# Order of TensorE's work in the even tiles of the attention blocks

## The chip, the cores and the metric

The kernel runs on one core of one Trainium2 chip. The metric is the device time of one execution in microseconds (us). Times come from repeated runs; the trace comes from one further execution, profiled by the hardware.

## What is computed

Three layers follow each other. Sparse attention: 2 batches, 8 heads, 576 tokens, head dimension 64, the softmax taken over the 32 largest scores of each row. A feed-forward layer on the 1152 tokens (model width 512, hidden width 2048) with a leaky ReLU whose slope is learned. A mixture of 8 experts, of which each token takes the best two.

```python
scores = scale * np.matmul(q, k.transpose(0, 1, 3, 2))
kth = np.partition(scores, -top_k, axis=-1)[..., -top_k:-top_k + 1]
attn = exp(where(scores >= kth, scores, -1e9) - max);  attn /= sum(attn)
x = np.matmul(attn, v)                                   # -> [1152, 512]
h = x @ w_in;  g = np.maximum(h, 0.0) + alpha * np.minimum(h, 0.0);  x2 = g @ w_out
# then gates, top 2 of 8 experts, and per expert relu(x2 @ w1[e]) @ w2[e]
```

## The kernel before

All is float32 in accuracy: large products are made of a high and a low part of each operand (`_high`, `_low`, `_parts`), so a product takes two or three passes of TensorE.

The 1152 tokens are cut in 9 **blocks** of 128 rows. A block has 8 **tiles**, one for each head h. Attention and feed-forward layer run together, as a pipeline over the tiles: while TensorE transposes the probabilities of tile h of block blk, it computes the scores of the tile 5 ahead (AHEAD), works on the feed-forward layer of block blk-1 (`mlp`) and finishes that of block blk-2 (`rest`). The feed-forward layer goes in 4 chunks of 512 hidden columns, chunk c of block j. `first_layer` makes a chunk of h in bank `ps_h`; ScalarE copies it to `h_sb` (`copy_h1`); TensorE turns it (`h_transpose`, four 128x128 transposes into `ps_t`); ScalarE takes the two ReLUs from `ps_t` (`relu_both`), GpSimd puts them together (`prelu`), ScalarE and GpSimd cut the result in a high and a low part (`high_g`, `low_g`), and `second_layer` multiplies it with w_out, 12 matmuls, into `ps_y`.

Each engine runs its own instruction list in order, and the lists are written by hand; semaphores are the only link. TensorE's list is made by `one_block`. Which tile does what is in small tables: `FIRST_AT` (first layer at h = 1, 3, 5, 7), `TURN_AT` (chunks 0, 1, 2 turned at h = 2, 4, 6), `REST_TURN_AT` (chunk 3 at h = 0 of the next block), `SECOND_AT` (chunk 0 at h = 6) and `REST_SECOND_AT` (chunks 1, 2, 3 at h = 0, 2, 4 of the next block). Turns and second layers thus lie in even tiles only.

What the functions of TensorE wait for:
- `prob_transpose` (L889, matmuls L896 and L898): GpSimd's masked probabilities, and ScalarE having emptied the banks.
- `score_tile` (L874, L865): the queries and that ScalarE has copied the scores of the tile before. In block 4 (MIXED), which holds rows of both batches, a tile's scores take 8 matmuls and not 4.
- `h_transpose` (L944, L952): `copy_h1` of its chunk (`act_h1`), and that `ps_t` is free.
- `prob_values` (L900, L912): `copy_prob_t` of this tile (`act_pt`), ScalarE's copy of the turned probabilities to SBUF. 20 small matmuls.
- `second_layer` (L955, L974): `low_g` of its chunk, which stands in GpSimd's list ahead of the probabilities of the same tile. For chunk 0 (h = 6) it also waits for `copy_x2_t` (`act_x2t`), by which ScalarE empties `ps_y` of the block before.
- `x_transpose` (L916, L921) at h = 1, `x2_transpose` (L979, L984) at h = 5 and `gates` (L987, L992) at h = 6.

ScalarE's list in an even tile is: `copy_h1` (L1251), `copy_prob_t` (L1221, L1222), at h = 6 `copy_x2_t` (L1318), the high parts of queries and g, `copy_scores` (L1161), `relu_both` (L1285, L1287), two exponentials (L1215). At h = 3 and 7 the list ends with `copy_o` (L1240, L1241), which waits for the `prob_values` of that tile; so at h = 0 and 4 `copy_h1` stands behind it.

After the 9 blocks a hand-written tail ends the feed-forward layer of blocks 7 and 8 and the routing, and then the expert phase runs, bound by TensorE, from about 504 us on.

Of the kernel before, what the change touches and what calls it, by code (L numbers as in the profile page):

```python
# [81 lines left out]
TURN_AT, REST_TURN_AT = {2: 0, 4: 1, 6: 2}, {0: 3}  # L82
# [3 lines left out]
SECOND_AT, REST_SECOND_AT = {6: 0}, {0: 1, 2: 2, 4: 3}  # L86
# [20 lines left out]
def chunk_of(j, c):  # L107

    return c if j % 2 == 0 else (c + 2) % CHUNKS


def wait(eng, sem, count):

    if not isinstance(count, int) or count > 0:
        eng.wait_ge(sem, count)


def moe_program(nc, q_in_rows, kt_in, v_in, v_tail, w_in, w_out, alpha, w_gates, noise, w1, w2, w_parts, x2_rows, x_sorted,
                out):
    with ExitStack() as ctx:  # L120
# [59 lines left out]
        def sb1(name, shape, dt=F32):  # L180
            return early.enter_context(nc.sbuf_tensor(name, shape, dt))
# [18 lines left out]
        rest = sb1("rest", [P, 2, SEQ])  # L200
# [660 lines left out]
        def _(pe):  # L861
# [12 lines left out]
            def score_tile(tile, h, blk, b):  # L874

                if h % 4 == 0:
                    pe.wait_ge(q_ready[h // 4], blk + 1)
                if isinstance(blk, int) and blk == 0:
                    keys_ready(0, h)
                wait(pe, act_scores, tile)  # L880
                if isinstance(blk, int) and blk == MIXED:
                    b, head = h // PAIRS, 2 * (h % PAIRS)
                    keys_ready(b, head + 1)
                    score_parts(h, b, head + 1)
                    score_parts(h, b, head, DIM).then_inc(pe_scores, 1)
                else:
                    score_parts(h, b, h).then_inc(pe_scores, 1)

            def prob_transpose(tile, h, blk):  # L889
                pe.wait_ge(pool_prob, tile + 1)  # L890
                wait(pe, act_pt, tile)
                if h == 0:
                    wait(pe, act_gate, blk - 2)
                for kt in range(KT):
                    if kt < KT - 1:
                        pe.transpose(ps_pt[:, kt * P:(kt + 1) * P], expo[:, h % 4, kt * P:(kt + 1) * P], ident[:, :])  # L896
                    else:
                        pe.transpose(ps_pt4[0:LASTK, 0:P], expo[:, h % 4, kt * P:SEQ], ident[:, :]).then_inc(pe_pt, 1)  # L898

            def prob_values(tile, h, blk, mixed_block, b):  # L900

                pe.wait_ge(act_pt, tile + 1)
                if h % 4 == 0:
                    wait(pe, act_o, 2 * blk + h // 4)
                if mixed_block and h >= PAIRS:
                    pe.wait_ge(v_in_second[h - PAIRS], 48)
                c = (h % 4) * VCOLS
                heads = (2 * (h % PAIRS), 2 * (h % PAIRS) + 1) if mixed_block else (h, h)
                for kt in range(KT):
                    n = P if kt < KT - 1 else LASTK  # L910
                    for lo, hi, head in ((0, DIM, heads[0]), (DIM, P, heads[1])):
                        mm = pe.matmul(ps_o[lo:hi, c:c + VCOLS], prob_t[0:n, h % 2, kt * P + lo:kt * P + hi],  # L912
                                       v[0:n, head, kt, :], start=(kt == 0), stop=(kt == KT - 1))
                mm.then_inc(pe_pv, 1)

            def x_transpose(j):  # L916
                pe.wait_ge(pool_x, 2 * j + 2)

                wait(pe, act_relu, 4 * j)
                for k in range(MK):  # L920
                    mm = pe.transpose(ps_t[:, k * P:(k + 1) * P], xf[:, k * P:(k + 1) * P], ident[:, :])  # L921
                mm.then_inc(pe_xt, 1)

            def first_layer(j, c, dst=ps_h[:, :], alone=False):
                if j == 0:
                    pe.wait_ge(pool_w_in_low, 2 * c + 2)
                elif c >= 2:
                    pe.wait_ge(w_in_back[c % 2], 16 * j)
                if c == 0:
                    pe.wait_ge(act_xt, j + 1)  # L930
                if not alone:
                    wait(pe, act_h1, 4 * j + c)
                for k in range(MK):
                    for b in range(2):
                        pe.matmul(dst, x_t[:, 0, k, :], w_in_parts[:, c % 2, b, k * 512:(k + 1) * 512],  # L935
                                  start=(k == 0 and b == 0), stop=False)
                if c == 0:
                    pe.wait_ge(dve_xt, j + 1)
                for k in range(MK):
                    mm = pe.matmul(dst, x_t[:, 1, k, :], w_in_parts[:, c % 2, 0, k * 512:(k + 1) * 512],  # L940
                                   start=False, stop=(k == MK - 1))
                mm.then_inc(pe_first, 1)

            def h_transpose(j, c, dst=ps_t, src=h_sb[:, :], banks=1):  # L944
                pe.wait_ge(act_h1, 4 * j + c + 1)

                if c == 0:
                    pe.wait_ge(dve_xt, j + 1)
                else:
                    pe.wait_ge(act_relu, 4 * j + c + 1 - banks)  # L950
                for k in range(4):
                    mm = pe.transpose(dst[:, k * P:(k + 1) * P], src[:, k * P:(k + 1) * P], ident[:, :])  # L952
                mm.then_inc(pe_ht1, 1)

            def second_layer(j, c):  # L955

                last = isinstance(j, int) and j == BLOCKS - 1
                if last:
                    pe.wait_ge(dve_g_low, c + 1)
                else:  # L960
                    pe.wait_ge(pool_g_low, 4 * j + c + 1)
                if j == 0:
                    if c == 2:
                        pe.wait_ge(dve_w_low, 2)
                    else:
                        pe.wait_ge(pool_w_low, (2, 4, 0, 6)[c])
                if c == 0:
                    wait(pe, act_x2, j)
                    if not last:
                        wait(pe, act_x2t, j)  # L970
                for k in range(4):
                    at = slice((4 * chunk_of(j, c) + k) * MODEL, (4 * chunk_of(j, c) + k + 1) * MODEL)
                    for a, w in ((0, w_out_high), (0, w_out_low), (1, w_out_high)):
                        mm = pe.matmul(ps_y[:, :], g_parts[:, c % 2, a, k * P:(k + 1) * P], w[:, at],  # L974
                                       start=(c == 0 and k == 0 and a == 0 and w is w_out_high),
                                       stop=(c == CHUNKS - 1 and k == 3 and a == 1))
                mm.then_inc(pe_second, 1)
# [18 lines left out]
            def one_block(blk, b, mixed_block=False, mlp=True, rest=True, last=False):  # L996
                for h in range(HEADS):
                    tile = HEADS * blk + h
                    prob_transpose(tile, h, blk)
                    if not (last and h + AHEAD >= HEADS):  # L1000
                        score_tile(tile + AHEAD, (h + AHEAD) % HEADS, blk + (h + AHEAD) // HEADS,
                                   1 if mixed_block and h + AHEAD >= HEADS else b)
                    if rest and h in REST_TURN_AT:
                        h_transpose(blk - 2, REST_TURN_AT[h])
                    if mlp and h == 1:
                        x_transpose(blk - 1)
                    if mlp and h in TURN_AT:
                        h_transpose(blk - 1, TURN_AT[h])
                    if h % 2 == 0 or h == 1:
                        prob_values(tile, h, blk, mixed_block, b)  # L1010
                    if mlp and h in FIRST_AT:
                        first_layer(blk - 1, FIRST_AT[h])
                    if mlp and h in SECOND_AT:
                        second_layer(blk - 1, SECOND_AT[h])
                    if rest and h in REST_SECOND_AT:
                        second_layer(blk - 2, REST_SECOND_AT[h])
                    if h % 2 and h != 1:
                        prob_values(tile, h, blk, mixed_block, b)
                    if rest and h == 5:
                        x2_transpose(blk - 2)  # L1020
                    if rest and h == 6:
                        gates(blk - 2)
# [13 lines left out]
            pe.wait_ge(ident_ready, 2)  # L1036
            pe.wait_ge(v_ready, 1)
            one_block(0, 0, mlp=False, rest=False)
            one_block(1, 0, rest=False)
            pe.wait_ge(small_in, 48)  # L1040
# [718 lines left out]
```

## Time and profile before

| | us |
|---|---|
| median of 3 runs | 758.64 |
| lowest and highest of them | 755.74 and 759.49 |
| the profiled execution, whole | 760.67 |
| its span, first to last instruction | 758.9 |

The profiled execution is 2.03 us above the median. In its span block 5 begins at 263.3 us, block 6 at 307.0, block 7 at 350.2 and block 8 at 393.3; a block in the steady part takes about 43.2 us. The trace gives for each instruction or run of like instructions its start and how long it was in flight. Matmuls overlap, so the distance from one start to the next is what an instruction costs TensorE, and its own duration is longer than that. A bracket at the end of a row is idle time of the engine ahead of it and what ended that. The releaser is sometimes named by the tile that another instruction of the same engine wrote.

### The profile page before, as it was taken

How to read it: one execution, taken by the hardware profiler on the slowest of the kernel's cores; microseconds unless marked ns; L12 is line 12 of the kernel's file. 1: busy time of each engine (PE TensorE's matmuls, PEld its weight loads, DVE VectorE, ACT ScalarE, POOL GpSimd, SP SyncE). 2: the span in 40 equal slices, each digit the busy share in tenths (PEclk: the TensorE clock that was granted, in tenths of full speed). 3: DMA queues.
4: the chain of work that ended last, by engine and by line, in shares of the span. 5: the costliest groups of instructions: out<-in, count | busy, mean ns of one | idle time of the engine just before them, and what ended most of it. 6: DMA issues, size and time to landing. Idle time of an engine off the chain costs nothing.

```text
span 758.9 us, 13760 instructions
## 1 busy us (share of the span) xinstructions
PE 664.5 (88%) x4660; PEld 564.7 (74%) x4660; DVE 521.5 (69%) x1103; ACT 465.2 (61%) x878; POOL 392.8 (52%) x435
## 2 busy tenths in 40 slices
PE   2467767999989999999999998369999999999993
PEld 2355656887867888888887777258989989989992
DVE  5799997888779989898989043454555554555520
ACT  5588866777887777777877545614554544535511
POOL 3488899678788677776787634400202202202112
PEclk9987998999999999999999999759999999999998
DMA  9759446643507536244644749380638448366222
GB/s 307 309 185 414 132 167 210 236 169 141 217 17 268 183 127 239 99 192 154 249 140 174 278 182 385 148 291 1 188 118 277 130 160 275 93 213 208 88 32 35
DMA packets 39607, 140.95 MB, mean 186 GB/s; under 512 B 10800, under 2 KB 11824, under 8 KB 35504
## 3 DMA queue, kind: packets, MB, share of 16 engines
q1 hardware_dynamic: 35168, 130.25, 47.5%
q0 software_dynamic: 4384, 9.98, 5.8%
q8 instruction: 32, 0.52, 0.3%
q14 instruction: 23, 0.19, 0.1%
HBM read 113.70 MB, written 45.73 MB: 210 GB/s over the span
## 4 chain that ended last, share of the span: by engine, by line
PE 70%; POOL 11%; DVE 5%; issue 4%; ACT 4%; DMA 4%; POOLq 0%; ACTq 0%; SPq 0%; DVEq 0%
PE bank L1125 12%; PE bank L974 11%; PE ps_scores L1111 9%; PE bank L935 7%; PE bank L1111 6%; PE bank L912 6%; PE bank L1130 4%; PE bank L940 3%; PE ps_scores L865 3%; POOL expo L1567 3%; PE bank L896 3%; DMA q_raw<-q_rows_dram 2%; PE bank L952 2%; DVE top L414 2%; PE bank L1093 1%
## 5 line engine op out<-in xcount | busy, mean ns | idle before, releaser
L1709 POOL DMA_INDIRECT out_dram<-ye,xe x24 | 42.8, 1783 | 219.1 <-ACT ye L1475 214.2
L414 DVE MAX8 top<-rest 128x8 f32<-128x576 f32 x216 | 152.2, 745 | 0.0
L1567 POOL TENSOR_TENSOR expo<-scores,expo 128x576 f32<-128x576 f32 x72 | 103.6, 1440 | 68.1 <-ACT scores L1195 68.0
L426 DVE MATCH_REPLACE8 rest<-top,rest 128x576 f32<-128x576 f32 x144 | 105.7, 741 | 0.0
L974 PE MATMUL bank<-w_out_high,g_parts 128*128 128x512 f32 x288 | 100.2, 410 | 0.0
L1125 PE MATMUL bank<-w_hi,he_t 128*128 128x512 f32 x256 | 91.9, 400 | 0.0
L604 DVE TENSOR_TENSOR w_lo<-raw,w_hi 128x1024 fp32r<-128x1024 f32 x64 | 77.8, 1225 | 19.5 <-ACT w_hi L1419 18.4
L912 PEld LDWEIGHTS bank<-v,prob_t 128*64 128x64 f32 (+1 forms) x1440 | 57.4, 145 | 30.2 <-ACT prob_t L1222 15.6
L912 PE MATMUL bank<-v,prob_t 128*64 128x65 f32 (+1 forms) x1440 | 73.1, 241 | 5.8 <-ACT prob_t L1222 5.8
L414 DVE MAX8 top<-scores 128x8 f32<-128x576 f32 x72 | 52.6, 746 | 33.7 <-ACT scores L1161 33.3
L935 PE MATMUL bank<-w_in_parts,x_t 128*128 128x512 f32 x272 | 71.2, 405 | 2.2 <-DMA w_in_parts<-w_parts_dram 2.2
L896 PE MATMUL bank<-ident,expo 128*128 128x128 f32 x288 | 47.9, 291 | 27.5 <-POOL expo L1567 26.2
L1111 PE MATMUL ps_scores<-xe_t,w_hi 128*128 128x320 f32 x320 | 71.8, 312 | 0.0
L865 PE MATMUL ps_scores<-k_parts,q_high 128*128 128x288 f32 (+1 forms) x160 | 55.4, 361 | 17.9 <-DVE q_low L471 8.1
L1221 ACT ACTIVATE prob_t<-bank 128x512 f32<-128x512 f32 x72 | 43.3, 601 | 43.2 <-PE bank L898 43.1
L1419 ACT CAST w_hi<-raw 128x1024 fp32r<-128x1024 f32 x64 | 66.2, 1044 | 0.2
L974 PEld LDWEIGHTS bank<-w_out_high,g_parts 128*128 128x128 f32 x288 | 54.8, 190 | 13.1
L1468 ACT ACTIVATE he_t<-ps_scores 128x320 fp32r<-128x320 f32 x40 | 17.5, 437 | 76.7 <-PE ps_scores L1111 76.7
L896 PEld LDWEIGHTS bank<-ident,expo 128*128 128x128 f32 x288 | 35.0, 149 | 35.6 <-POOL expo L1567 21.7
L935 PEld LDWEIGHTS bank<-w_in_parts,x_t 128*128 128x128 f32 x272 | 50.1, 192 | 11.9 <-DMA w_in_parts<-w_parts_dram 2.4
L650 DVE SCALAR_TENSOR_TENSOR he_t<-ps_scores,he_t 128x64 fp32r<-128x64 f32 x80 | 22.2, 319 | 53.2 <-ACT he_t L1468 53.2
L1111 PEld LDWEIGHTS ps_scores<-xe_t,w_hi 128*128 128x128 f32 x320 | 55.4, 191 | 2.1
(192 smaller groups left out, 1606.3 us busy)
## 6 DMA issues: line engine op xcount, KB each, us to landing
w_in_parts<-w_parts_dram SPq DMA_DIRECT2D x16, 2048.0 KB, 7.9
raw<-w_dram SPq DMA_DIRECT2D x64, 512.0 KB, 10.8
x_sorted_dram<-x_sorted_dram SPq DMA_DIRECT2D x7, 2570.0 KB, 10.9
w_parts_dram<-w_in_parts SPq DMA_DIRECT2D x4, 2048.0 KB, 10.1
q_raw<-q_rows_dram SPq DMA_DIRECT2D x18, 256.0 KB, 5.0
xe<-x_sorted_dram SPq DMA_DIRECT2D x8, 514.0 KB, 4.6
w_in_raw<-w_in_dram SPq DMA_DIRECT2D x4, 1024.0 KB, 11.0
w_out_raw<-w_out_dram SPq DMA_DIRECT2D x4, 1024.0 KB, 15.8
```

Source lines behind the costliest of these rows:

```text
L414: nc.vector.max(dst, src).then_inc(chain if r < ROUNDS - 1 else dve_top, 1)
L426: nc.vector.match_replace(rest[:, k, :], top[:, (n + k) % 4, 8 * r:8 * r + 8], src, LOWEST).then_inc(chain, 1)
L604: nc.vector.tensor_tensor(w_lo[par][:, at], raw[par][:, at], w_hi[par][:, at].bitcast(F32), ALU.subtract).then_inc(dve_wl, 1)
L865: mm = pe.matmul(ps_scores[0:to, n, 0:HALF], part[:, n_q, 0:to], k_parts[:, k_slot(b, h), n * HALF:(n + 1) * HALF], start=(a == 0), stop=( ...
L896: pe.transpose(ps_pt[:, kt * P:(kt + 1) * P], expo[:, h % 4, kt * P:(kt + 1) * P], ident[:, :])
L912: mm = pe.matmul(ps_o[lo:hi, c:c + VCOLS], prob_t[0:n, h % 2, kt * P + lo:kt * P + hi], v[0:n, head, kt, :], start=(kt == 0), stop=(kt == ...
L935: pe.matmul(dst, x_t[:, 0, k, :], w_in_parts[:, c % 2, b, k * 512:(k + 1) * 512], start=(k == 0 and b == 0), stop=False)
L974: mm = pe.matmul(ps_y[:, :], g_parts[:, c % 2, a, k * P:(k + 1) * P], w[:, at], start=(c == 0 and k == 0 and a == 0 and w is w_out_high), ...
L1111: mm = pe.matmul(h_bank[m % 3][:, 0:GROUP], w[:, k, at], xe_t[:, a, k, :], start=(k == 0 and a == 0 and w is w1_hi), stop=(k == MK - 1 and ...
L1125: mm = pe.matmul(y_bank[t][:, :], he_t[:, m, at:at + P], w[:, m, :], start=(m == 0 and a == 0 and w is w2_hi), stop=(m == EK - 1 and a == 1))
L1419: nc.scalar.copy(w_hi[par][:, at], raw[par][:, at]).then_inc(act_wh, 1)
L1567: nc.gpsimd.tensor_tensor(expo[:, n % 4, :], scores[:, n % SBUFS, :], expo[:, n % 4, :], ALU.mult).then_inc(pool_prob, 1)
```

## The change

Only TensorE's order within a tile changes. In the even tiles of blocks with feed-forward work it was: transposes of the probabilities, scores, turn of a feed-forward chunk, product with the values, second layer. It becomes: transposes, turn, scores, second layer, product with the values. Odd tiles, the order on the other engines, all waits and all instructions stay as they are. In block 0 there is no feed-forward work and the order is the same; in block 1 chunks 0 to 2 are turned and one second layer runs. `gates` at h = 6 stays behind everything.

```diff
@@ one_block of TensorE @@
                     prob_transpose(tile, h, blk)
+                    if rest and h in REST_TURN_AT:
+                        h_transpose(blk - 2, REST_TURN_AT[h])
+                    if mlp and h in TURN_AT:
+                        h_transpose(blk - 1, TURN_AT[h])
                     if not (last and h + AHEAD >= HEADS):
                         score_tile(tile + AHEAD, (h + AHEAD) % HEADS, blk + (h + AHEAD) // HEADS,
                                    1 if mixed_block and h + AHEAD >= HEADS else b)
-                    if rest and h in REST_TURN_AT:
-                        h_transpose(blk - 2, REST_TURN_AT[h])
+                    if mlp and h in SECOND_AT:
+                        second_layer(blk - 1, SECOND_AT[h])
+                    if rest and h in REST_SECOND_AT:
+                        second_layer(blk - 2, REST_SECOND_AT[h])
                     if mlp and h == 1:
                         x_transpose(blk - 1)
-                    if mlp and h in TURN_AT:
-                        h_transpose(blk - 1, TURN_AT[h])
                     if h % 2 == 0 or h == 1:
                         prob_values(tile, h, blk, mixed_block, b)
                     if mlp and h in FIRST_AT:
                         first_layer(blk - 1, FIRST_AT[h])
-                    if mlp and h in SECOND_AT:
-                        second_layer(blk - 1, SECOND_AT[h])
-                    if rest and h in REST_SECOND_AT:
-                        second_layer(blk - 2, REST_SECOND_AT[h])
```

## Rows read from the trace of the kernel before

**Rows 1.** The page: busy time by engine, and the chain by engine.
```profile
PE 664.5 (88%) x4660; PEld 564.7 (74%) x4660; DVE 521.5 (69%) x1103; ACT 465.2 (61%) x878; POOL 392.8 (52%) x435
...
PE 70%; POOL 11%; DVE 5%; issue 4%; ACT 4%; DMA 4%; POOLq 0%; ACTq 0%; SPq 0%; DVEq 0%
```

**Rows 2.** Windows: length, busy us of PE, PEld, DVE, ACT, POOL, granted clock, DMA, GB/s.
```profile
216.00:259.00 43.00, 40.37 (x334) 33.22 (x332) 35.25 (x74) 32.63 (x69) 33.10 (x41) 1.00 0.53 176
...
302.00:345.00 43.00, 43.00 (x360) 35.43 (x360) 39.49 (x84) 33.09 (x70) 32.47 (x40) 1.00 0.48 176
```

**Rows 3.** Waits from 300 to 400 us: who waited for whom, us, times, longest.
```profile
POOL expo L1567 <- ACT scores L1195: 20.3, 9, 2.7
...
DVE top L414 <- ACT scores L1161: 6.1, 5, 1.6
```

**Rows 4.** Timeline of PE, block 6, h = 0: start, us in flight, instruction.
```profile
307.00 0.66 PE L896 MATMUL bank<-ident,expo 128*128 128x128 f32 x4
...
307.52 0.38 PE L865 MATMUL ps_scores<-k_parts,q_high 128*128 128x288 f32 x1
...
308.30 0.66 PE L952 MATMUL bank<-ident,h_sb 128*128 128x128 f32 x4
...
312.69 0.60 PE L896 MATMUL bank<-ident,expo 128*128 128x128 f32 x4
```

**Rows 5.** Timeline of ACT, and one row of POOL, block 6.
```profile
307.11 0.26 ACT L1240 ACTIVATE den<-bank,least 128x4 f32<-128x4 f32 x1 [1.49 <-PE bank L912]
...
307.65 0.59 ACT L1251 COPY h_sb<-bank 128x512 f32<-128x512 f32 x1
...
318.27 0.59 ACT L1251 COPY h_sb<-bank 128x512 f32<-128x512 f32 x1 [1.31 <-PE bank L940]
...
340.59 0.57 ACT L1318 COPY x<-bank 128x512 f32<-128x512 f32 x1
...
308.83 1.42 POOL L1567 TENSOR_TENSOR expo<-scores,expo 128x576 f32<-128x576 f32 x1
```

**Rows 6.** Timeline of PE, block 6: h = 2 (318.07) and h = 6 (339.19).
```profile
318.07 0.60 PE L896 MATMUL bank<-ident,expo 128*128 128x128 f32 x4
...
318.53 0.38 PE L865 MATMUL ps_scores<-k_parts,q_high 128*128 128x288 f32 x1
...
323.44 0.60 PE L896 MATMUL bank<-ident,expo 128*128 128x128 f32 x4
...
339.19 0.60 PE L896 MATMUL bank<-ident,expo 128*128 128x128 f32 x4
...
344.55 0.96 PE L992 MATMUL bank<-gates_w,x 128*128 128x16 f32 x8
```

**Rows 7.** Timeline of PE in the odd tile before: scores, first layer, product with the values.
```profile
302.66 0.38 PE L865 MATMUL ps_scores<-k_parts,q_high 128*128 128x288 f32 x1
...
303.27 1.99 PE L935 MATMUL bank<-w_in_parts,x_t 128*128 128x512 f32 x8
305.10 1.08 PE L940 MATMUL bank<-w_in_parts,x_t 128*128 128x512 f32 x4
306.12 0.95 PE L912 MATMUL bank<-v,prob_t 128*64 128x65 f32 x20
```

**Rows 8.** Timeline of PE, block 8, h = 4: the turn, with no scores ahead of it.
```profile
415.08 0.66 PE L952 MATMUL bank<-ident,h_sb 128*128 128x128 f32 x4 [0.42 <-ACT h_sb L1251]
```

**Rows 9.** Timeline of PE, and one row of ACT, blocks 3 and 4.
```profile
212.28 0.59 ACT L1221 ACTIVATE prob_t<-bank 128x512 f32<-128x512 f32 x1
...
215.37 0.66 PE L896 MATMUL bank<-ident,expo 128*128 128x128 f32 x4 [0.72 <-POOL expo L1567]
...
219.13 0.66 PE L952 MATMUL bank<-ident,h_sb 128*128 128x128 f32 x4 [1.39 <-ACT h_sb L1251]
...
225.72 0.66 PE L921 MATMUL bank<-ident,x 128*128 128x128 f32 x4 [0.41 <-POOL x L1586]
```

**Rows 10.** Timeline of PE, block 2: eight matmuls of the first layer behind idle time.
```profile
130.44 3.78 PE L935 MATMUL bank<-w_in_parts,x_t 128*128 128x512 f32 x8
```

## The prediction

> **What bounds the kernel now.** I read the page first: TensorE is busy 88% of the span, VectorE 69%, and 70% of the chain that ended last lies on TensorE [rows 1]. An average over the stages says little, so next the windows, each about a block long: from 302 to 345 us TensorE's matmuls fill 43.00 of 43.00 us, VectorE 39.5, ScalarE 33, GpSimd 32.5, at a granted clock of 1.00 [rows 2]. Then the waits: from 300 to 400 us GpSimd waits 20.3 us in 9 places for ScalarE, VectorE 6.1 us for scores [rows 3]; TensorE waits for nobody by more than a fraction of a microsecond. So from block 2 on the others follow TensorE. Last the timeline, where the reader should look at the distance from start to start, for this is what a matmul costs in a packed queue. As TensorE takes its list in order, a wait put in it delays all behind it, and in a packed block nothing gives that back.
>
> **The change, part by part.** No instruction is added or removed, so only two things can move time: waits, and the price of one kind of matmul following another.
>
> *The wait of the turn.* `h_transpose` needs `copy_h1` to be done. In block 6 at h = 0 the transposes of the probabilities start at 307.00 and the scores at 307.52 [rows 4]. ScalarE begins `copy_o` only at 307.11, after TensorE's last product with the values, and then copies h from 307.65 to 308.24 [rows 5]; the turn starts at 308.30, 0.06 us after it [rows 4]. Between 307.52 and 308.30 TensorE now does the scores. After the change the turn is wanted at 307.52, the scores stand behind it, and TensorE is idle for 0.78 us. ScalarE's start hangs on TensorE, not on a clock of its own, so this returns in each block at h = 0 and, by the same list, at h = 4. Block 8 shows the new order already: at h = 4 there are no scores, and the turn waits 0.42 us of visible idle for the copy [rows 8].
>
> *The sum of one such tile.* From the start of the turn at 308.30: turn to scores 0.46 (as transposes to scores, 318.07 to 318.53 [rows 6]); scores to a large matmul 0.61 (302.66 to 303.27); 12 large matmuls at (305.10 - 303.27) / 8 = 0.229, or 2.75; large matmul to product with the values 0.10 (306.12 less 305.10 less 4 x 0.229) [rows 7]; that product 0.88 (306.12 [rows 7] to 307.00 [rows 4]); and the next transposes cost 0.06 more behind it (0.52 to the scores at h = 0 [rows 4], 0.46 at h = 2 [rows 6]). Together 4.86, so the next tile is where it would be with a start at 313.16. It was 312.69 [rows 4]: **+0.47 us** at h = 0 and h = 4. Of the idle time of 0.78 the old order had 0.17 already (the scores, 0.61, did not fill it), and the remaining 0.14 are cheaper changes from one kind of matmul to the next (the turn is no longer followed by small products, nor these by large ones).
>
> *At h = 2* ScalarE starts the copy at 318.27, as soon as the first layer of h = 1 is done, and ends at 318.86 [rows 5]. Turn at 318.92, plus 4.86 gives 323.78 against 323.44 [rows 6]: **+0.34 us**.
>
> *At h = 6* h has long been copied, but the second layer of chunk 0 waits for `copy_x2_t`, which ends at 340.59 + 0.57 = 341.16 [rows 5]. Now the product with the values stands ahead of it and hides that. After the change transposes, turn and scores are done about 1.6 us behind 339.19 [rows 6], at 340.8; the second layer starts at 341.22, and with 2.75, 0.10 and 0.88 `gates` starts at 344.95 against 344.55 [rows 6]: **+0.40 us**. This one comes from moving the second layer, the others from moving the turn.
>
> *What moves at no cost.* The product with the values comes some 3 us later; its readers in even tiles are only the freeing of `prob_t`, two tiles off, and at block 4 loads of v that are used four tiles later; the SyncE queue waits behind them for events of h = 1 and 3, which are later anyway. If that cover were gone a load would delay the tile by what it is late, which no row shows; I take nothing. The scores come later, but ScalarE copies them only at 309.81 by its own list, behind the queries and g, and they are done at about 309.6 by the sum above. The second layer's `low_g` stands in GpSimd's list ahead of the probabilities on which the tile's first transposes have waited, so it never waits for GpSimd.
>
> *All blocks.* A whole steady block costs 0.47 + 0.34 + 0.47 + 0.40 = 1.68. Nothing in it absorbs that: GpSimd has the next tile's probabilities at 308.83 + 1.42 = 310.25 [rows 5], 2.4 us before TensorE takes them at 312.69 [rows 4]. Blocks 5, 6, 7: 5.0. For the others I put the same prices, with what differs. Block 2: its h = 0 lies before idle time for GpSimd and is free, the other three give 1.2. Block 3: h = 0 is lost in a wait for GpSimd at h = 1; h = 2 gives 0.34; h = 4, where 8 score matmuls had filled the old wait of 0.17, 0.64; h = 6 is lost, since from 203 us on ScalarE is behind with the keys of the second batch (it turns to the probabilities of h = 7 at 212.28, 3 us after TensorE began them) and TensorE's next tile waits 0.72 for GpSimd anyway [rows 9]. Block 4: at h = 0 the turn waits for ScalarE until 219.13 in either order, but 8 score matmuls (0.61 and 4 x 0.13) now stand behind it, about +1.0 with the cheaper changes taken off, of which 0.6 go into the old wait of `x_transpose` for GpSimd (0.41 visible [rows 9]): 0.44; with the other three 1.65. Block 8: 0.47 + 0.34, then h = 4 without scores -0.14 (same wait [rows 8], cheaper changes), h = 6 +0.40: 1.1. Blocks 0 and 1 are set by GpSimd with TensorE idle: 0. Sum 1.2 + 1.0 + 1.65 + 5.0 + 1.1 = **9.9 us**. The tail and the expert phase start from TensorE's end of block 8 and only shift.
>
> The sum is made against the profiled execution (760.67, span 758.9), which lies 2.03 above the median; I add it to the median: 758.64 + 9.9 = **768.5 us**.
>
> **A rule against this.** TensorE's matmuls cover each window whole, while its weight loads fill 35.43 of 43.00 us, 82% [rows 2]. The Trainium skill (Perfetto Trace Analysis, Identifying the Most-Contended Engine) says that matmul busy time doesn't tell how near TensorE is to its limit and that the busy share of weight loads does. By that rule, as I read it, a block has 7.6 us open, 1.7 us of waits fit in, and the time would stay. No run here has shown that yet.
>
> **The rivals.** (a) *Not slower: TensorE has slack that the rows hide.* Matmuls in flight overlap, so "busy" may cover idle slots; if the waits fall into such slots, only the cheaper changes remain, between 0 and 0.14 for each of 27 even tiles, 0 to 3.8 us; the middle gives 756.7. For it: weight loads leave 18% of a window. Against it: the starts of large matmuls stand 0.229 us apart with no holes [rows 7], and block 8's turn does show idle time [rows 8]. It decides only if a wait of 0.78 at h = 0 costs under 0.3. Chance 0.07. (b) *Half of it is absorbed*, because another engine, above all VectorE with 39.5 of 43 us [rows 2], sets part of the pace: about +5, 763.6. Against it VectorE itself waits for scores [rows 3]. Chance 0.12. (c) *The clock falls.* Behind idle time in block 2 eight large matmuls take 3.78 us in flight [rows 10] against 1.99 [rows 7]: half clock (1.2 GHz). If the new gaps brought one such stretch to each of 7 blocks, at 1.8 us or more, 13 us come on top: 781. Against it: idle times of 1.39 and 0.41 us in block 4 [rows 9] left the granted clock of the window from 216 us at 1.00 [rows 2]. Chance 0.04. That the change doesn't do what it says is excluded where the list is simply rewritten.
>
> **How the numbers follow.** Forecast 0.77, (a) 0.07, (b) 0.12, (c) 0.04. The forecast's own bounds: the step from turn to scores may be 0.1 off, 0.3 us a block; and blocks 2 to 4 could give from 1 to 6 us instead of 3.8; so 764 to 772. The same idle times in block 2 may shift the low-clock stretch there by up to 2 us either way. To leave no more than 2 in 10 out I go from 761.5, which takes in most of (b), to 773. A run of this kernel can tell a change from none at about 0.5%, 3.8 us. Faster 0.03, same 0.12 ((a) and the low part of (b)), slower 0.85.
>
> **What would show it.** In the new timeline, the turn at h = 0, 2 and 4 of blocks 5 to 7 is preceded by an idle bracket for ScalarE's copy of h, its start still 1.3 us behind the tile's first transpose at h = 0 and 4, and the tiles are 0.3 to 0.5 us longer; at h = 6 the bracket stands before the second layer, for ScalarE's copy of the turned x2. A steady block lasts 44.8 to 45.0 us against 43.2. VectorE's and GpSimd's waits grow by as much. I am wrong if the blocks keep 43.2 us with these brackets there (rival a), if the block is longer by under 1 us (rival b), or if the clock in rows of blocks 5 to 7 is under 1.00 (rival c); also if `copy_h1` comes sooner because ScalarE's list runs less behind than I think.

## The result, and the profile after

| | us |
|---|---|
| before, median of 6 runs | 758.75 (755.24 to 759.49) |
| changed kernel, median of 6 runs | 769.08 (767.37 to 771.25) |
| ratio, 95% interval | 1.0145 (1.0123 to 1.0167) |
| profiled execution of the changed kernel, whole and span | 769.32 and 767.6 |

The change costs 10.3 us by the medians. A second set of the same kernel, run beside some of the experiments, gave 769.31 us and a ratio of 1.0129 (1.0094 to 1.0165).

First the page of the changed kernel, busy time and chain, which answer to [rows 1]:

```profile
PE 663.6 (86%) x4660; PEld 560.3 (73%) x4660; DVE 522.3 (68%) x1103; ACT 466.0 (61%) x878; POOL 393.0 (51%) x435
...
PE 69%; POOL 10%; ACT 6%; DVE 5%; issue 5%; DMA 4%; ACTq 0%; POOLq 0%; SPq 0%; DVEq 0%
```

The busy time of TensorE's matmuls, VectorE, ScalarE and GpSimd moved by less than 1 us each, so the loss isn't more work. ScalarE's share of the chain went from 4% to 6%: it now sets the end in places. The windows answer to [rows 2] (same columns):

```profile
216.00:259.00 43.00, 39.10 (x294) 32.19 (x295) 31.49 (x65) 30.87 (x66) 30.61 (x37) 0.92 0.46 150
...
302.00:345.00 43.00, 41.40 (x346) 33.22 (x344) 37.97 (x81) 32.49 (x69) 30.59 (x39) 1.00 0.47 178
```

In the steady window TensorE has 1.60 us of idle time where it had none, and every engine behind it does less in the same 43 us. The first row holds block 4: there the granted clock is 0.92 and no longer 1.00. The waits from 300 to 400 us answer to [rows 3]:

```profile
POOL expo L1567 <- ACT scores L1195: 25.0, 9, 3.4
...
DVE top L414 <- ACT scores L1161: 8.0, 7, 1.8
...
PE bank L952 <- ACT h_sb L1251: 2.0, 4, 0.5
```

VectorE's wait grew from 6.1 to 8.0 us and GpSimd's from 20.3 to 25.0: they follow, they don't set the pace. TensorE's wait for the copy of h is new in this list.

The timeline of block 6 (start, us in flight, instruction) has the three places of the forecast. At h = 0, which answers to [rows 4]:

```profile
312.31 0.66 PE L896 MATMUL bank<-ident,expo 128*128 128x128 f32 x4
...
313.61 0.66 PE L952 MATMUL bank<-ident,h_sb 128*128 128x128 f32 x4 [0.53 <-ACT h_sb L1251]
314.02 0.38 PE L865 MATMUL ps_scores<-k_parts,q_high 128*128 128x288 f32 x1
...
314.63 0.39 PE L974 MATMUL bank<-w_out_high,g_parts 128*128 128x512 f32 x1
...
317.47 0.95 PE L912 MATMUL bank<-v,prob_t 128*64 128x65 f32 x20
318.35 0.66 PE L896 MATMUL bank<-ident,expo 128*128 128x128 f32 x4
```

The turn starts 1.30 us behind the tile's first transpose, as before (307.00 to 308.30 [rows 4]), but the scores are no longer ahead of it. The tile takes 6.04 us against 5.69. At h = 2 (323.78) and h = 6 (345.59), which answer to [rows 6]:

```profile
323.78 0.60 PE L896 MATMUL bank<-ident,expo 128*128 128x128 f32 x4
324.62 0.66 PE L952 MATMUL bank<-ident,h_sb 128*128 128x128 f32 x4
...
329.37 0.66 PE L896 MATMUL bank<-ident,expo 128*128 128x128 f32 x4
...
345.59 0.60 PE L896 MATMUL bank<-ident,expo 128*128 128x128 f32 x4
...
347.70 0.47 PE L974 MATMUL bank<-w_out_high,g_parts 128*128 128x512 f32 x1 [0.44 <-ACT x L1318]
...
350.63 0.95 PE L912 MATMUL bank<-v,prob_t 128*64 128x65 f32 x20
351.51 1.07 PE L992 MATMUL bank<-gates_w,x 128*128 128x16 f32 x8
352.42 0.64 PE L896 MATMUL bank<-ident,expo 128*128 128x128 f32 x4
```

h = 2 takes 5.59 us (5.37 before); it waits too, but so little that matmuls in flight cover it and no bracket shows. h = 6 takes 6.83 us (6.16 before), and the bracket names the copy of the turned x2. Block 7 begins at 357.26, so block 6 takes 44.95 us and not 43.19: +1.76.

### The profile page after: what moved, and what is told of

Its sections match the earlier page's. It is cut to its first block, busy times and chain, and to the rows that moved or that the text cites. A ratio compares the mean times of both kernels' runs of the same rounds, so it can differ in the third digit from the quotient of the medians.

```text
span 767.6 us, 13760 instructions
## 1 busy us (share of the span) xinstructions
PE 663.6 (86%) x4660; PEld 560.3 (73%) x4660; DVE 522.3 (68%) x1103; ACT 466.0 (61%) x878; POOL 393.0 (51%) x435
## 4 chain that ended last, share of the span: by engine, by line
PE 69%; POOL 10%; ACT 6%; DVE 5%; issue 5%; DMA 4%; ACTq 0%; POOLq 0%; SPq 0%; DVEq 0%
PE bank L1125 11%; PE bank L974 11%; PE ps_scores L1111 9%; PE bank L935 7%; PE bank L1111 6%; PE bank L912 6%; PE bank L1130 4%; PE ps_scores L865 4%; PE bank L940 3%; POOL expo L1567 3%; DMA q_raw<-q_rows_dram 2%; PE bank L896 2%; PE bank L952 2%; DVE top L414 2%; ACT h_sb L1251 2%
## 5 line engine op out<-in xcount | busy, mean ns | idle before, releaser
L974 PE MATMUL bank<-w_out_high,g_parts 128*128 128x512 f32 x288 | 97.9, 402 | 3.2 <-ACT x L1318 3.2
L974 PE MATMUL bank<-w_out_low,g_parts 128*128 128x512 f32 x144 | 57.1, 396 | 0.0
```

## Block 4: idle time that let the clock fall

At h = 0 of block 4 ScalarE is late with the keys of the second batch: its copy of h starts only at 217.63 us. The changed kernel, to be set beside [rows 9], first that row of ScalarE, then TensorE:

```profile
217.63 0.58 ACT L1251 COPY h_sb<-bank 128x512 f32<-128x512 f32 x1
...
214.51 0.66 PE L896 MATMUL bank<-ident,expo 128*128 128x128 f32 x4
...
218.27 1.11 PE L952 MATMUL bank<-ident,h_sb 128*128 128x128 f32 x4 [2.99 <-ACT h_sb L1251]
...
221.10 0.63 PE L974 MATMUL bank<-w_out_high,g_parts 128*128 128x512 f32 x1
221.53 0.63 PE L974 MATMUL bank<-w_out_low,g_parts 128*128 128x512 f32 x1
...
225.42 0.95 PE L912 MATMUL bank<-v,prob_t 128*64 128x65 f32 x20
226.30 0.66 PE L896 MATMUL bank<-ident,expo 128*128 128x128 f32 x4
```

The idle time was 1.39 us, with 8 score matmuls ahead of it; now they stand behind it and it is 2.99 us in one piece. After it the large matmuls start 0.43 us apart (221.10 to 221.53) and not 0.229: the engine runs at 1.2 GHz (the granted clock from 218.3 to 224.4 us is 0.51). The last four of the 12 are at full clock again; together they take 4.32 us (221.10 to 225.42) and not 2.83. The tile takes 11.79 us against 8.16; the next one gives 0.56 back (5.95 against 6.51), as its wait for GpSimd has gone.

## The experiments

Each kernel was timed against the kernel before on the same chip; the sets lie on three chips, with medians of before of 759.30 us (each half alone; the waits taken away), 758.39 (early copy in the old order, best of both, block 4, the second trace of the changed kernel) and 756.44 (the second copy alone). So ratios, and not times, are compared from one set to another. "A steady block" is the distance from the first transpose of block 6 to that of block 7. My theory: the loss is TensorE's wait for two ScalarE copies, one uncovered by each half of the change. Rival: the loss lies in the new neighbourhood of matmuls, whatever they wait for.

**Each half alone.** The turn moved ahead of the scores, nothing else:

```diff
                     prob_transpose(tile, h, blk)
+                    if rest and h in REST_TURN_AT:
+                        h_transpose(blk - 2, REST_TURN_AT[h])
+                    if mlp and h in TURN_AT:
+                        h_transpose(blk - 1, TURN_AT[h])
                     if not (last and h + AHEAD >= HEADS):
...
-                    if rest and h in REST_TURN_AT:
-                        h_transpose(blk - 2, REST_TURN_AT[h])
...
-                    if mlp and h in TURN_AT:
-                        h_transpose(blk - 1, TURN_AT[h])
```

> Only the turn is moved ahead of the scores; the second layer stays behind the product with the values. Theory (the cost is TensorE waiting for two ScalarE copies, each set free by one half of the change): the wait for the copy of h costs 0.4 us at h = 0 and 4 and 0.3 us at h = 2, h = 6 costs nothing, so a steady block is 1.0 to 1.1 us longer than before (44.2 to 44.3 us), and h = 0 of block 4, where ScalarE is late and TensorE's clock fell in the changed kernel, adds some 3 us. Whole: 7 to 9 us over before, ratio 1.009 to 1.012. Rival (the price is the new neighbourhood of matmuls, paid in every even tile by both halves alike): half of the loss, ratio 1.007, and h = 6 is longer too.

Measured 766.35 us, ratio 1.0085 (1.0048 to 1.0121). The wait is there and h = 6 is untouched (342.52 to 348.69 is 6.17 us; before 6.16):

```profile
309.08 0.66 PE L896 MATMUL bank<-ident,expo 128*128 128x128 f32 x4
...
310.37 0.66 PE L952 MATMUL bank<-ident,h_sb 128*128 128x128 f32 x4 [0.53 <-ACT h_sb L1251]
...
342.52 0.60 PE L896 MATMUL bank<-ident,expo 128*128 128x128 f32 x4
...
348.69 0.64 PE L896 MATMUL bank<-ident,expo 128*128 128x128 f32 x4
...
353.53 0.66 PE L896 MATMUL bank<-ident,expo 128*128 128x128 f32 x4
```

A steady block is 353.53 - 309.08 = 44.45 us, 1.26 more than before; I had expected 1.0 to 1.1. The tiles h = 0, 2 and 4 are longer by 0.47, 0.34 and 0.47 us. The ratio lies under the range that I gave, but its interval reaches from below the rival's 1.007 to above mine; the ratio doesn't tell the two apart, the tiles do.

The second layer moved ahead of the product with the values, the turn left behind the scores:

```diff
                     if mlp and h in TURN_AT:
                         h_transpose(blk - 1, TURN_AT[h])
+                    if mlp and h in SECOND_AT:
+                        second_layer(blk - 1, SECOND_AT[h])
+                    if rest and h in REST_SECOND_AT:
+                        second_layer(blk - 2, REST_SECOND_AT[h])
...
                     if h % 2 == 0 or h == 1:
                         prob_values(tile, h, blk, mixed_block, b)
...
-                    if mlp and h in SECOND_AT:
-                        second_layer(blk - 1, SECOND_AT[h])
-                    if rest and h in REST_SECOND_AT:
-                        second_layer(blk - 2, REST_SECOND_AT[h])
```

> Only the second layer is moved ahead of the product with the values; the turn stays behind the scores. Theory: h = 0, 2 and 4 become 0.1 to 0.2 us shorter each, for cheaper changes between kinds of matmul; h = 6 becomes 0.6 to 0.7 us longer, because the second layer waits for the copy of the turned x2. A steady block 43.2 to 43.4 us; whole 0 to 2 us over before, ratio 1.000 to 1.003. Rival (both halves alike): ratio 1.007.

Measured 761.91 us, ratio 1.0032 (1.0005 to 1.0060), just above the range that I gave and with an interval that leaves out the rival's 1.007. Block 6 begins at 308.58 and block 7 at 352.16:

```profile
308.58 0.66 PE L896 MATMUL bank<-ident,expo 128*128 128x128 f32 x4
...
340.49 0.60 PE L896 MATMUL bank<-ident,expo 128*128 128x128 f32 x4
...
342.61 0.47 PE L974 MATMUL bank<-w_out_high,g_parts 128*128 128x512 f32 x1 [0.44 <-ACT x L1318]
...
347.33 0.63 PE L896 MATMUL bank<-ident,expo 128*128 128x128 f32 x4
...
352.16 0.66 PE L896 MATMUL bank<-ident,expo 128*128 128x128 f32 x4
```

h = 6 takes 347.33 - 340.49 = 6.84 us, with the same bracket; a steady block is 43.58 us, +0.39, since the other tiles got shorter. The halves give 1.26 + 0.39 = 1.65 of the 1.76 us. They aren't alike, against the rival: one costs at h = 0, 2 and 4, the other at h = 6.

**The waits taken away, the order kept.** In the changed kernel ScalarE copies h ahead of `copy_o` at h = 3 and 7. The last line of the cut stands in the tail, where the copy is no longer needed, as h = 7 has made it:

```diff
-                    if rest and h in REST_TURN_AT:
-                        copy_h1(blk - 2, REST_TURN_AT[h])
-                    if mlp and h in TURN_AT:
+                    if mlp and h in TURN_AT and h != 4:
                         copy_h1(blk - 1, TURN_AT[h])
...
+                    if mlp and h % 4 == 3:
+                        copy_h1(blk - 1, FIRST_AT[h])
                     if h % 4 == 3:
                         copy_o(blk, h)
...
-            copy_h1(j - 1, 3)
```

> The changed kernel, with ScalarE's copy of h placed ahead of its copy of the attention output at h = 3 and 7, so that it waits for the first layer and not for the product with the values. Theory: the idle time before the turn at h = 0 and 4 vanishes, each such tile 0.6 to 0.7 us shorter than in the changed kernel, h = 2 and h = 6 unchanged; a steady block 43.6 to 43.8 us; whole 761 to 763 us, ratio 1.002 to 1.005. Rival (the loss is in the order of the matmuls, not in the wait): stays at 1.0145.

Measured 762.08 us, ratio 1.0027 (0.9995 to 1.0059). TensorE at h = 0 of block 6:

```profile
305.55 0.66 PE L896 MATMUL bank<-ident,expo 128*128 128x128 f32 x4
...
306.15 0.60 PE L952 MATMUL bank<-ident,h_sb 128*128 128x128 f32 x4
...
310.84 0.66 PE L896 MATMUL bank<-ident,expo 128*128 128x128 f32 x4
```

The turn follows at once; the tile takes 5.29 us and not 6.04, with the same order of matmuls. A steady block is 43.45 us (block 7 at 349.00), a little under the expected 43.6.

In block 4 the wait isn't taken away. There ScalarE is late with the keys as well; the turn at h = 0 still waits 2.57 us, and the tile takes 10.18 us (8.16 before):

```profile
215.97 0.66 PE L952 MATMUL bank<-ident,h_sb 128*128 128x128 f32 x4 [2.57 <-ACT h_sb L1251]
```

Then `copy_x2_t` too, ahead of `copy_prob_t` at h = 6:

```diff
+                    if rest and h == 6:
+                        copy_x2_t(blk - 2, xf, ps_y)
                     copy_prob_t(tile, h)
...
-                    if rest and h == 6:
-                        copy_x2_t(blk - 2, xf, ps_y)
```

> As the kernel with the early copy of h, and ScalarE's copy of the turned x2 also ahead of the copy of the probabilities at h = 6. Theory: the wait before the second layer at h = 6 vanishes too, 0.6 to 0.7 us a block; a steady block 43.0 to 43.1 us, only h = 2 still waits; whole 755 to 759 us, ratio 0.996 to 1.000. Rival (the loss is in the order of the matmuls): stays at 1.0145.

Measured 754.54 us, ratio 0.9941 (0.9907 to 0.9976), a little better than expected. h = 6 takes 6.15 us (338.18 to 344.33), and a steady block 349.16 - 306.40 = 42.76 us:

```profile
306.40 0.66 PE L896 MATMUL bank<-ident,expo 128*128 128x128 f32 x4
...
338.18 0.60 PE L896 MATMUL bank<-ident,expo 128*128 128x128 f32 x4
...
344.33 0.64 PE L896 MATMUL bank<-ident,expo 128*128 128x128 f32 x4
...
349.16 0.66 PE L896 MATMUL bank<-ident,expo 128*128 128x128 f32 x4
```

So the order of the matmuls as such isn't what costs: the same order, with two ScalarE copies placed for it, takes 0.6% less than the kernel before. That fells the rival. It doesn't make the order a gain; the early copy in the old order, below, tells what the copy alone is worth. Block 4 keeps its tile of 10.18 us here too.

The second copy alone, with the turn's wait left in:

> The changed kernel with only the copy of the turned x2 ahead of the copy of the probabilities at h = 6. Theory: h = 6 becomes 6.15 us and not 6.83, the other tiles keep their waits; a steady block 44.25 to 44.3 us and not 44.95; whole 4 to 5 us under the changed kernel, ratio 1.008 to 1.010. Rival (the wait at h = 6 moves to the product with the values, which now waits for the later copy of the probabilities): h = 6 stays at 6.8 us.

Measured 765.99 us, ratio 1.0127 (1.0095 to 1.0160). In the trace the step is as forecast: h = 6 of block 6 takes 6.15 us (343.44 to 349.59) and a steady block 44.25 us. The ratio is above the 1.008 to 1.010 that I expected, with an interval that just takes in the upper end. Against the changed kernel's 1.0145 and 1.0129 it is lower by 0.0018 and 0.0002, at most 1.4 us and not 4 to 5. (That 765.99 us is 3 us under the changed kernel's medians says little: before was 2 to 2.3 us faster on this chip, too.) The place of the loss at h = 6 is shown, its size in the whole time is not confirmed by this run.

**The early copy in the old order:**

> The kernel before, in its old order of TensorE, with ScalarE's copy of h ahead of its copy of the attention output at h = 3 and 7. Theory: it takes away the small waits that the old order had at the turn (0.2 to 0.3 us at h = 0 and 4, 0.8 us in the tiles behind the mixed block); a steady block 42.6 to 42.7 us; whole 2 to 5 us under before, ratio 0.994 to 0.997.

Measured 754.66 us, ratio 0.9935 (0.9906 to 0.9963), a little under what I expected:

```profile
303.52 0.66 PE L896 MATMUL bank<-ident,expo 128*128 128x128 f32 x4
...
346.20 0.65 PE L896 MATMUL bank<-ident,expo 128*128 128x128 f32 x4
```

A steady block is 42.68 us. At h = 0 of block 5, behind the mixed block, the gain is 0.50 us (6.24 to 5.74) and not 0.8. The kernel with both copies early has 42.76 us and 0.9941, so, as far as the runs can tell, its whole gain over before has nothing to do with the change: the copy of h was behind `copy_o` in the kernel before, too. And not all of this copy's gain lies in the turn's wait. From the start of h = 7 of block 8 to the end of the span the four kernels with the early copy of h take 324.3 to 325.6 us, the other eight traces 327.0 to 333.1. Which part of the tail gives that was not traced.

**The best of both:** the second layer moved, the turn left behind the scores, both copies early.

> Order transposes, scores, turn, second layer, product with the values (only the second layer moved), with both ScalarE copies early. Theory: no wait is left at any even tile, at h = 2 the scores cover the copy of h, and the cheaper neighbourhood of the second layer is kept; a steady block 42.2 to 42.5 us; whole 6 to 9 us under before, ratio 0.988 to 0.993. Rival (what the earlier kernel with both copies early gained comes from the turn's place): no better than that kernel, 0.994.

Measured 751.25 us, ratio 0.9900 (0.9873 to 0.9926), 1.0% faster than before. A steady block:

```profile
302.89 0.66 PE L896 MATMUL bank<-ident,expo 128*128 128x128 f32 x4
...
345.41 0.66 PE L896 MATMUL bank<-ident,expo 128*128 128x128 f32 x4
```

This is 42.52 us, 0.67 less than before and just above what was expected. In blocks 5 to 8 TensorE has no bracket at all; at h = 0 of block 4 the turn still waits 0.97 us. Against the rival a steady block is 0.24 us shorter than in the kernel with the changed order and both copies early, and 0.16 shorter than with the early copy in the old order. The ratios (0.9900 against 0.9941 and 0.9935) say the same, but their intervals overlap.

**Block 4.** The old place of the turn in one single tile:

```diff
+                    late = isinstance(blk, int) and blk == MIXED and h == 0
-                    if rest and h in REST_TURN_AT:
+                    if rest and h in REST_TURN_AT and not late:
                         h_transpose(blk - 2, REST_TURN_AT[h])
...
+                    if late:
+                        h_transpose(blk - 2, REST_TURN_AT[h])
```

> The changed kernel, but at h = 0 of block 4 alone the turn stays behind the 8 score matmuls, so that TensorE isn't idle for 3 us in one piece. Theory (that one idle time let TensorE's clock fall, and the slow stretch behind it costs more than the wait): the tile is 8.0 to 8.3 us and not 11.8, no slow stretch there; whole 3 us under the changed kernel, ratio 1.010 to 1.011. Rival (the tile's loss is the wait alone, and the slow clock is chance): the tile is 1 us shorter, ratio 1.013 or more.

Measured 767.91 us, ratio 1.0111 (1.0083 to 1.0138). The trace:

```profile
217.50 0.66 PE L896 MATMUL bank<-ident,expo 128*128 128x128 f32 x4
...
221.26 0.66 PE L952 MATMUL bank<-ident,h_sb 128*128 128x128 f32 x4 [1.40 <-ACT h_sb L1254]
...
225.48 0.66 PE L896 MATMUL bank<-ident,expo 128*128 128x128 f32 x4
...
232.20 0.60 PE L896 MATMUL bank<-ident,expo 128*128 128x128 f32 x4
```

The tile takes 7.98 us and not 11.79, the idle time is 1.40 again, and no matmul runs slow. The next tile takes 6.72 us and not 5.95, as it waits for GpSimd again, so the pair goes from 17.74 to 14.70 us. That is 3.0 us against the changed kernel's first trace, and 1.85 against its second one (16.55 us, below). The medians are 1.4 us apart (769.31 for the changed kernel beside it) and not the 3 that I forecast, and the ratios (1.0111 against 1.0129) point the same way with intervals that overlap. So the step in the tile is shown, its size in the whole time is not.

That the low clock comes with the long idle time, and is no chance here, all 12 traces bear out. At this tile the turn waited 2.57 to 2.99 us in one piece in six of them (the changed kernel twice, the turn alone moved, the second copy alone, and the two with the changed order and the early copy of h): in all six TensorE ran at 1.2 GHz behind it, and the tile took 10.18 to 11.79 us. In the other six the wait was 0.97 to 1.40 us, and the tile took 7.57 to 8.17 us at full clock.

**A second trace of either kernel.**

> The changed kernel once more, for a second trace. Theory: steady blocks 44.95 us again and idle time of 3 us with a low clock at h = 0 of block 4 again, since both follow from the order. Where the low clock of block 2 and of the tail fall is chance, and may differ by some 3 us between two executions of one kernel.

Its time stands above. Steady blocks are 44.95 us again. Block 4 again has 2.99 us of idle time at h = 0, and slow matmuls behind it, for a shorter while: the tile takes 10.60 us, not 11.79:

```profile
213.93 0.65 PE L896 MATMUL bank<-ident,expo 128*128 128x128 f32 x4
...
217.68 0.66 PE L952 MATMUL bank<-ident,h_sb 128*128 128x128 f32 x4 [2.99 <-ACT h_sb L1251]
...
224.53 0.66 PE L896 MATMUL bank<-ident,expo 128*128 128x128 f32 x4
```

> The kernel before once more, for a second trace. Theory: steady blocks 43.2 us again; the tile h = 1 of block 2 (10.1 us in the first trace, 7.3 and 6.5 in two traces of the changed kernel) and the tail differ by up to 3 us from the first trace, since where the clock falls there is chance and not the order. Rival: 10.1 us again, and the changed order then gains 3 us there.

One execution, 755.32 us. A steady block is 43.18 us. Its tile h = 1 of block 2:

```profile
123.94 0.66 PE L896 MATMUL bank<-ident,expo 128*128 128x128 f32 x4 [0.99 <-POOL expo L1567]
...
131.22 0.60 PE L896 MATMUL bank<-ident,expo 128*128 128x128 f32 x4
```

That tile takes 7.28 us, where the first trace of the same kernel has 10.11, with large matmuls at half clock [rows 10]. That fells the rival. Over the 12 traces it took 7.28 to 10.11 us with the turn behind the scores and 6.51 to 10.21 with the turn ahead of them. The 6.51 are no gain: h = 0 is 0.76 us longer there. The two tiles together took 13.9 to 16.8 us in either order, so the low clock adds up to 2.9 us here, by chance. At h = 1 of block 3 it did so too in two traces (8.95 and 8.89 us, with the second layer alone moved and with the early copy in the old order; 7.26 in the kernel before).

## Why the prediction was right

Forecast 768.5 us and 9.9 us over before; measured 769.08 and 10.3. The mechanism is as told: two waits for ScalarE copies, at the tiles named, added undiminished in packed blocks; a steady block of 44.95 us lies in the forecast 44.8 to 45.0. That the whole came out within 0.6 us is luck in part, as the table shows. Price by price:

| place | forecast | measured |
|---|---|---|
| h = 0 and 4, steady blocks | +0.47 | +0.40 (0.35 in the tile, 0.05 in the next) |
| h = 2 | +0.34 | +0.28 (0.22 and 0.06) |
| h = 6 | +0.40 | +0.67 |
| a steady block | 1.68 | 1.76 |
| blocks 0 and 1 | 0 | 0.9, against the first trace of before -0.1 |
| blocks 2 and 3 | 2.2 | 2.1 |
| block 4 | 1.65 | 4.4, in the second trace 3.2 |
| blocks 5 to 7 | 5.0 | 5.3 |
| block 8 | 1.1 | 1.3 |
| expert phase and tail | 0 | 0 (327.1 us from the end of h = 6 of block 8 to the span's end, 327.0 before; 329.5 and 328.5 in the other trace of each) |

The rows on blocks 0 to 4, block 8 and the tail compare the changed kernel's first trace with the second one of before, in which block 2 happens to be as fast as in the changed kernel.

- *The wait of the turn* came out to 0.01 us: 1.30 behind the first transpose. The step from turn to scores is 0.41 (313.61 to 314.02), not the 0.46 that I had borrowed from transposes. The parts of the price come out of the tiles with the early copy: the wait costs 0.75 (6.04 against 5.29) and not 0.78, the old order had 0.26 of it already (5.69 against 5.43, early copy in the old order) and not 0.17, and the cheaper neighbours give 0.14 (5.43 against 5.29), as forecast.
- *h = 6* was the worst-sized of the repeated terms. The wait ended as forecast within 0.1 (347.70 is 2.11 behind 345.59; I had 2.03), but the 12 matmuls and the change behind them took 2.93 and not 2.85, and `gates` then takes 0.91 to the next transposes, where it took 0.80 behind large matmuls. I had ended the tile's sum at the start of `gates`, one step too soon.
- *What is absorbed* came as told. Block 3 at h = 0 is 0.37 longer and the next tile 0.36 shorter; h = 6 is 0.77 longer and h = 7 is 0.78 shorter.
- *Block 4* is the term that failed. I said that the turn waits for ScalarE "until 219.13 in either order" and priced the scores behind it, 1.0. That the same scores had cut the idle time to 1.39 us, and that it would be 2.99 without them, I did not draw; so rival (c), the clock, which I took for 0.04 because 1.39 us had not lowered it, came true in this one tile. Beyond the 9.0 us that the tile would take at full clock (3.76 + 0.41 + 1.14 + 2.83 + 0.88), the low clock cost 2.8 us in the first trace and 1.6 in the second. The wait alone was sized fairly: at full clock the tile would be 0.86 longer and the next one gives 0.56 back, 0.3 against the forecast 0.44.
- *Rival (a)* fell: each wait shows in full, though weight loads filled only 82% of a window. With the waits they fill 33.22 of 43 us, 77%, and the block is 1.76 us longer. The Trainium skill (Perfetto Trace Analysis, Identifying the Most-Contended Engine) takes that share, beside the kernel's FLOPs against the peak, as the measure of how near TensorE is to its limit; here it did not tell whether a wait is hidden. The starts, 0.229 us apart without holes, did.
- *Rival (b)* fell with the longer waits of VectorE and GpSimd.

By stage the terms on blocks 2 to 8 make 13.1 us, or 11.9 with the changed kernel's second trace for block 4, and not the 10.3 of the medians. The interval of the ratio, 1.0123 to 1.0167, is 9.3 to 12.7 us, so the 11.9 lies in it and the 13.1 just outside. What blurs the comparison is the chance in each execution: the two traces of before are 5.35 us apart (760.67 and 755.32), of which block 2 with its low clock has 2.9, the tail 1.5 and blocks 0 and 1 the rest, and the changed kernel's 769.32 is 8.65 us above the one and 14.0 above the other. The mis-sized block 4 thus does not show clearly in the medians and that the forecast of 9.9 came so near to the 10.3 is luck in part. Whether something else gives a part of it back stays open.

## What to carry to other kernels

Ahead of a reordering on a packed in-order engine, write beside each moved instruction when its operand is ready, counted from a fixed point of the tile: what lay between was cover, and the loss is what it covered, less what cheaper neighbours give. A wait on a copy that itself waits for this engine returns in each tile and shrinks by nothing; look for its cause in the other engine's list, where moving one copy ahead of one that waits for something later gained 0.65% here without touching TensorE's order. And where a moved block had split an idle stretch, add up the idle time that is now in one piece.

## What the runs showed of the hardware that I had not expected

- TensorE fell to 1.2 GHz behind 2.99 us of idle time in both traces of the changed kernel, and for a different length of time in each (the tile took 11.79 and 10.60 us); at the same place it did so behind 2.57 us in two traces of other kernels, and behind 1.39 and 1.40 us it did not. In block 2, with the same idle time of 1.66 us ahead of `x_transpose`, it was slow in one trace of before and not in the other: 10.11 and 7.28 us for the same tile of the same kernel.
- `gates`, eight small matmuls, costs 0.91 us from its start to the next transposes behind the product with the values, and 0.80 behind the large matmuls of the second layer.
